# Moving seven weight transfers of the expert loop from the SyncE queue to the ScalarE queue

## What is computed

```python
x = attention(q, k, v)                     # 2304 tokens x 512
do_compute = x @ w_skip > 0                # the other tokens keep x
e_idx = argmax(xc @ w_gate)                # one of 8 experts per token
for e in range(8):
    h = maximum(xc[mask] @ w1[e], 0.0)     # w1: 512 x 1024
    y[mask] = gate_w[mask] * (h @ w2[e])   # w2: 1024 x 512
out[do_compute] = xc + y
h = out @ w_in                             # w_in: 512 x 2048
g = h * clip(h + 3, 0, 6) / 6
result = g @ w_out                         # w_out: 2048 x 512
```

## Time and profile before

| | |
|---|---|
| time, median of 3 runs | 666.27 us (664.95 to 668.8) |
| profiled execution, span | 667.5 us |
| TensorE busy | 632.4 us (95% of the span) |
| expert loop in the profile | about 125 to 273 us |
| mean granted clock | 0.990 |

### The profile page before, as it was taken

The page is one execution under the profiler, slowest core; times in us unless marked ns, Lnnn a source line. Parts: engine busy times, 40 slices in busy tenths (PEclk is TensorE's granted clock), DMA queues, the critical chain, the costliest instruction groups (busy, mean ns, idle before and its releaser), DMA issues.

```text
span 667.5 us, 17127 instructions
## 1 busy us (share of the span) xinstructions
PE 632.4 (95%) x6454; PEld 549.9 (82%) x6454; DVE 396.2 (59%) x1070; ACT 321.5 (48%) x674; POOL 91.6 (14%) x160
## 2 busy tenths in 40 slices
PE   7899986798799989999999999999999999999998
PEld 6688874676678868898898898888888988888896
DVE  2678886311111122497766679777777788777743
ACT  3798884111112122664454556654455475444433
POOL 4333452431101011100000002100000021000000
PEclk9999999799989999999999999999999999999999
DMA  9876848498878785622222222623222233122102
GB/s 157 179 175 151 204 125 329 135 326 282 274 288 307 241 313 186 198 64 80 79 80 64 63 64 66 205 79 80 80 63 64 64 110 111 64 63 64 33 0 95
DMA packets 114132, 93.56 MB, mean 140 GB/s; under 512 B 62893, under 2 KB 90033, under 8 KB 114065
## 3 DMA queue, kind: packets, MB, share of 16 engines
q1 hardware_dynamic: 97696, 56.10, 30.9%
q10 hardware_dynamic: 12720, 25.58, 11.0%
q0 software_dynamic: 3648, 11.00, 4.4%
HBM read 80.08 MB, written 12.97 MB: 139 GB/s over the span
## 4 chain that ended last, share of the span: by engine, by line
PE 84%; DMA 4%; DVE 4%; issue 3%; ACT 1%; POOLq 1%; another core or an unknown queue 1%; POOL 0%; SPq 0%; DVEq 0%
PE bank L1093 30%; PE av L1035 27%; PE bank L994 7%; PE av L1006 7%; DMA xin<-x_rows 3%; PE bank L807 2%; PE av L851 2%; PE bank L792 2%; PE bank L867 2%; DVE sm L1460 1%; DMA x_rows<-yo,yrow 1%; PE av L965 1%; PE bank L897 1%; PE av L1022 1%
## 5 line engine op out<-in xcount | busy, mean ns | idle before, releaser
L1093 PE MATMUL bank<-o_hi,g_lo 128*128 128x512 f32 x288 | 114.0, 396 | 0.0
L1093 PE MATMUL bank<-o_hi,g_hi 128*128 128x512 f32 x288 | 113.9, 395 | 0.0
L1093 PE MATMUL bank<-o_lo,g_hi 128*128 128x512 f32 x288 | 113.5, 394 | 0.0
L1035 PE MATMUL av<-xc_hi,w_hi 128*128 128x384 f32 x344 | 89.5, 341 | 0.0
L1035 PE MATMUL av<-xc_hi,w_lo 128*128 128x384 f32 x344 | 88.3, 337 | 0.0
L1035 PE MATMUL av<-xc_lo,w_hi 128*128 128x384 f32 x344 | 88.2, 337 | 0.0
L1764 DVE TENSOR_TENSOR g_lo<-act,g_hi 128x384 fp32r<-128x384 f32 x96 | 53.4, 556 | 43.6 <-ACT g_hi L1328 40.4
L994 PEld LDWEIGHTS bank<-xeT,w1s 128*64 128x64 f32 x2176 | 69.2, 139 | 10.7 <-issue 8.4
L994 PE MATMUL bank<-xeT,w1s 128*64 128x64 f32 x2176 | 71.1, 224 | 6.4 <-issue 5.9
L1328 ACT CAST g_hi<-act 128x384 fp32r<-128x384 f32 x96 | 49.4, 515 | 51.4 <-DVE act L1757 49.4
L1035 PEld LDWEIGHTS av<-xc_hi,w_hi 128*128 128x128 f32 x344 | 63.0, 188 | 13.2 <-DVE act L1757 0.9
(11 more groups left out here) (182 smaller groups left out, 945.0 us busy)
## 6 DMA issues: line engine op xcount, KB each, us to landing
w1s<-in_moe_w ACTq DMA_DIRECT2D x6, 2048.0 KB, 10.1
w2s<-in_moe_w ACTq DMA_DIRECT2D x6, 2048.0 KB, 17.1
wor<-in_moe_w_out SPq DMA_DIRECT2D x24, 512.0 KB, 3.8
wir<-in_moe_w_in SPq DMA_DIRECT2D x24, 256.0 KB, 4.2
wir<-in_moe_w_in SPq DMA_DIRECT2D x48, 128.0 KB, 4.1
qraw<-in_q SPq DMA_DIRECT2D x36, 128.0 KB
vnow<-in_v SPq DMA_DIRECT2D x36, 128.0 KB, 3.6
kraw<-in_k SPq DMA_DIRECT2D x34, 128.0 KB
```

What stands on the lines that cost most here:

```text
L1035: last = pe.matmul(into[:, 0:GN], a[it % 2][:, W_AT[w], c, :], b[:, X_AT[x], c, :], start=(n == 0 and fresh), stop=(n == 3 * XQ * len(pair ...
L1093: last = pe.matmul(bank[tile][:, :], a[c][:, i * P:(i + 1) * P], b[it % 2][:, units(it)[c], :], start=(p == 0 and c in (0, 2) and n == 0), ...
```

## The change

Pair 2 (2 x 2 MB) is issued by ScalarE, right behind pair 1 and a wait for `s_ready`. The first MLP weights are issued by ScalarE at the ends of e = 2, 3, 4 and 5, behind the expert matrices that it issues there. SP issues nothing but rows in the expert loop.

```diff
+        def load_w_in(eng, it):      # as SP's own before, with the engine as an argument
+        def load_w_out(eng, it):
...
                 if e == 1:
                     sp.wait_ge(s_ready, 2 * RD0)
-                    load_w1(sp, 2, s_wp1[2])
-                    load_w2(sp, 2, s_wp2[2])
                 elif e == 2:
                     sp.wait_ge(s_padp, 16 * (NE - 2))
-                elif e == 4:
-                    load_w_in(0)
-                elif e == 5:
-                    load_w_out(0)
-                    load_w_in(1)
-                elif e == 7:
-                    load_w_out(1)
...
                     load_w1(sc, 1, s_wp1[1])
                     load_w2(sc, 1, s_wp2[1])
+                    sc.wait_ge(s_ready, 2 * RD0)
+                    load_w1(sc, 2, s_wp1[2])
+                    load_w2(sc, 2, s_wp2[2])
                     first = 1
...
                     load_w1(sc, e + 3, s_wp1[e % 3])
                     load_w2(sc, e + 3, s_wp2[e % 3])
+                if e == 2:
+                    load_w_in(sc, 0)
+                elif e == 3:
+                    load_w_out(sc, 0)
+                elif e == 4:
+                    load_w_in(sc, 1)
+                elif e == 5:
+                    load_w_out(sc, 1)
```

More of the change, by code:

```diff
@@ L498, in load_gate @@
             eng.dma_start(wg[:, :, NE:NE + 1], moe_w_skip.rearrange("(c p a) -> p c a", p=P, a=1), allow_slow_non_contiguous=True).then_inc(s_wg, 16)
+        def load_w_in(eng, it):
+            if it >= 2:
+                eng.wait_ge(s_wlo, it - 1)
+            quarters = moe2_w_in.rearrange("(k c p) (u f m) -> p u f k c m", k=2, c=XQ, u=2, f=FP)
+            chunks = moe2_w_in.rearrange("(c p) (u f m) -> p u f c m", c=DC, u=2, f=FP)
+            eng.dma_start(wir[it % 2][:, 1:3, :, :].rearrange("p k c m -> p (k c) m"), chunks[:, 0, it % FP, :, :]).then_inc(s_wir[it % 2], 16)
+            for h in range(2):
+                eng.dma_start(wir[it % 2][:, 3 * h, :, :], quarters[:, 1, it % FP, h, :, :]).then_inc(s_wir[it % 2], 16)
+        def load_w_out(eng, it):
+            if it >= 2:
+                eng.wait_ge(s_olo, it - 1)
+            halves = moe2_w_out.rearrange("(u f p) n -> p u f n", u=2, f=FP)
+            eng.dma_start(wor[it % 2][:, :, :], halves[:, :, it % FP, :]).then_inc(s_wor[it % 2], 16)
         def turned_in(T):
@@ L541, in load_rows @@
                     sp.dma_start(xin[h * ET:(h + 1) * ET, :], x_rows[row, h * HW:(h + 1) * HW]).then_inc(s_xin, 16)
[L543 to L556, removed]
             sp.sem_inc(s_ready, RD0)
@@ L623, in _ @@
                 if it + 2 < NQ:
-                    load_w_in(it + 2)
+                    load_w_in(sp, it + 2)
                 if it + 2 < NQ:
-                    load_w_out(it + 2)
+                    load_w_out(sp, it + 2)
                 if it == 0:
```

## The result

The changed kernel takes 692.01 us, the median of 4 runs (690.81 to 695.54), where the kernel before takes 666.46 us (664.95 to 668.8) beside it: a ratio of 1.0376, with a 95% interval of 1.0333 to 1.0418. I had forecast 662.9 us and given "slower" 9%. It is 25.6 us slower. (The title counts seven weight transfers. They are six loads, and ten transfers: `w_in(0)` and `w_in(1)` are three each, one of 256 KB and two of 128 KB.) The span of its profiled execution is 689.2 us, against 667.5 us before, and the mean granted clock is 0.972, against 0.990.

What follows compares the result with a forecast made beforehand. The prediction took TensorE's products as the bound, with idle waits for rows queued behind weights on SP's queue. Gains of 2.15 and 1.2 us, say 3.4, gave a median of 662.9 us, 8 in 10 from 661.0 to 667.0.

Steps and rivals of the forecast that it cites:

- part 3: ScalarE's added issues at the ends of e = 2 to 5: about 0.5 us each, hidden, no effect on the time.
- part 1: Pair 2 leaves SP's queue: the 2.65 us wait for rows 5 becomes 0.5 us, a gain of 2.15 us.
- Rival 2: After tile 0, ScalarE's queue lacks room for four 2 MB transfers and holds the issue: 669.2, up to 676 us; 6%.
- Part 2: 1 MB of MLP weights no longer ahead of rows 13: the 1.32 us stall goes to 0.1, a gain of 1.2 us.
- Rival 1: Stores of tiles 1 and 2 take 7.36 us, so a gain of 2.15 us becomes 0.9: 664.2 us; 25%.
- Rival 3: Rows in the loop are late with any traffic, whichever queue it is on; loop loses 4.7 us: 671.0 us; 3%.
- Rivals 4 and 5: First-tile code fetch: tile 5's meets the weight stream, 666.3 us (6%); or tile 6's shortens, down to 659.5 us (5%).

Runs made afterwards that it cites:

- e2_mlp_act: Kernel before, with only the MLP weights moved to ScalarE, behind the expert matrices; pair 2 stays with SP: 684.15 us, ratio 1.0232.
- g3_small_first: Kernel before, with only the MLP weights moved to ScalarE, issued ahead of the expert matrices of their place: 654.56 us, ratio 0.9995.
- h1_change_no_hold: Changed kernel, but `w2` of pair 2 issued by SP one expert later, behind rows 5, and MLP weights ahead of the pairs: 663.56 us, ratio 0.9966.
- e1_pair2_act: Kernel before, with only pair 2 moved to ScalarE; MLP weights stay with SP: 672.78 us, ratio 1.0054.
- g1_before_again: The kernel before, unchanged, profiled once more on a faster chip: 654.52 us, ratio 0.9987.
- e3_sp_later: Kernel before, all loads still on SP, but pair 2 one expert later, behind rows 5, and `w_in(1)` behind rows 13: 668.60 us, ratio 1.0024.
- f3_w2_4k_after: Changed kernel, with `w2` read in runs of 4 KB instead of 2 KB and `w1` columns picked in steps of two: 671.51 us, ratio 1.0294.
- f4_w2_4k_best: Kernel before, with pair 2 on ScalarE, `w2` in runs of 4 KB, MLP weights on SP with `w_in(1)` one expert later: 657.67 us, ratio 1.0068.

## Why the prediction was wrong

**The step that failed** is part 3, "What ScalarE takes on", with its "One issue costs about 0.5 us" and "Hidden, with 0.8 us to spare", and the same step inside part 1, "Two issues follow, 0.38 and 0.53 us like the others". I took the duration of an issue as a property of the instruction. It is one of the queue's state. The three issues of `w_in(0)`, which I put at 1.5 us, took 9.5 us (0.60 and 8.87), the fourth issue of part 1 took 9.15 us instead of 0.53, and the single `w_out(0)` 3.13 us instead of 0.4. The rows that I took 0.5 us from were SP's issues into a nearly empty queue.

**Rival 2** had the mechanism and, at its one place, nearly the size: "tile 1's second product starts 6.3 us late", measured 6.55 us. It was wrong in three ways. I gave it 6%. I looked at it at tile 1 alone, while issues stand behind a pair in three more places; the waits there are 7.18, 1.34 and 7.85 us. And I priced the wait without the clock, which adds 6.7 us. With these the rival would have read 666.5 + 22.9 + 6.7 - 3.4 = 692.7 us, and 692.01 was measured. What I held against it, "issue times elsewhere don't follow the backlog", was true of the trace and proved nothing. The 0.75 us at 178.06 are no sign either way, since an issue with one matrix alone ahead of it took longer:

```profile
169.92 1.09 ACTq L324 DMA_DIRECT2D w2s<-in_moe_w  x1
```

The trace had no issue behind more than two unmoved matrices (at 178.06 some 90 descriptors for each DMA engine, counted as in the last part of this section; the fourth issue after tile 0 had 131), so it could not exclude the rival. That called for a chance of some 30%, not 6%.

**Part 1** was right in its mechanism and is hidden under the loss: no wait for rows 5 in the kernel after. The wait stays in the runs that leave pair 2 on SP's queue in its old place (2.87 us in `e2_mlp_act`, 3.12 in `g3_small_first`) and is gone in those that take it away. With the holds removed, TensorE waits 0.58 us for rows and 0.84 us for VectorE in that stretch (`h1_change_no_hold`), where I had put 0.5 for all of it. **Part 2** is not shown: the wait for rows 13 is gone in the kernel after, but also in `e1_pair2_act` and `g1_before_again`, which keep what I took for its cause. Both together were forecast at 3.4 us; `h1_change_no_hold` has 2.4 us (from 4.6 to none by its interval).

**Rival 1**, stores that give the gain back, shows in that 0.84 us and no further. **Rival 3** is excluded: rows on a queue of their own beside a full stream of 2 and 4 KB runs are never the wait in the kernel after. **Rivals 4 and 5** stay open: the idle time at tile 6 is 3.42 us before, 2.87 after, 0.67 in `e3_sp_later` and absent in `g1_before_again`, and nothing that I changed is seen to control it. That it is a fetch of code is my reading; no run tested it.

**The rule of the Trainium skill** that I set against part 1, that the issuing engine only changes the issue time ("DMA: Bandwidth & Descriptors", section "Issuing engines are not separate DMA queues"), gives no change, and the traces differ both ways. The engine that issues decides who is held, 9.15 us here; and rows on a queue of their own passed weights that they did not pass on a shared one (the earlier trace rows against the 4.11 us of `e3_sp_later`).

**What stays open** is the limit itself. One transfer puts a number of descriptors on each of the 16 DMA engines: 33 for `w1` (512 runs of 4 KB over 16, and one for the end), 65 for `w2`. A pair, 98, shows in the trace of before as 1,568 packets on ScalarE's queue, 98 for each engine. Ahead of the fourth issue after tile 0 stand 33 + 65 + 33 = 131 of them. The fourth issue returned at 143.05, 10.75 us after the first issue. In that time ScalarE's queue had taken this (packets, MB, share of 16 engines):

```profile
q10 hardware_dynamic: 628, 2.30, 65.0%
```

That is 39 descriptors for each engine, so 92 of the 131 were left, and 4.0 of the 6.3 MB. By the same reckoning some 82 of 131 were left at 210.41, when the first small transfer was taken; 73 of 99 in `f3_w2_4k_after`, 76 of 99 in `f4_w2_4k_best`, and 80 of 98 where the third issue returned in `e2_mlp_act`. Against these stand issues that were not held: the third one in the kernel after, taken in 0.60 us behind the same 98, and the `w2s` at 187.60 in `g3_small_first`, taken in 0.53 us behind 103. So a fixed count of descriptors left does not settle it by itself, and I have no reading that fits all rows.

## What to carry to other kernels

An engine that issues a DMA can be held by it: before moving an issue onto an engine that computes, count the descriptors that already stand in that engine's queue, and treat a trace that never shows such a backlog as no evidence that it is free. If it must be there, put the small transfers ahead of the large ones, give a transfer long runs (which cost the rows on the other queue time here), or share a burst between two queues. That an engine with nothing else to do is the one to hold is an argument, not a result: no run here held SP. And price a wait of TensorE's of several microseconds with the slower clock behind it, here some 9 us for 7.

## What the runs showed of the hardware

- On ScalarE's queue an issue takes 0.37 to some 1.5 us, or up to 9.19 us (`e1_pair2_act`), by what stands ahead of it and not by its own size: one of 128 KB was held for 7.40 us.
- The count that holds it follows the runs, not the bytes: 9.15 us with `w2` in runs of 2 KB, 6.00 us with 4 KB (on a faster chip), 1.09 us with 16 KB for the fourth of the same four transfers. A held issue returned with 73 to 92 descriptors for each DMA engine still ahead of it.
- Long runs have their own price for others: rows beside runs of 16 KB took 10.0 to 11.6 us from issue to use, beside 2 and 4 KB 7.1 us.
- After TensorE had stood idle for 6.55 to 7.85 us, the clock was granted at 0.50 for a while, and the next product took 5.49 to 6.41 us instead of 3.67; in `f3_w2_4k_after` 6.60 us after a wait of 3.30. After a wait of 1.34 us it took 3.67 us. In the kernel before, the mean granted clock was 0.72 over the 6 us from 184 on, behind the idle 3.42 us of tile 6, and 1.00 in the 5 us from 165 on, behind the wait of 2.65 us.
- The same program took 667 and 653 us on different chips, 2%, several times the gain in question here.
